# Moving the taps' subtraction of the maximum from VectorE to GpSimd

## The reference

```
w = exp(weight_gen - max over the 7 taps)          # [4, 4096, 8 heads, 7]
w = w / (sum over taps + 1e-9)
x1[s] = sum_k w[s, h, k] * x_pad[s + k]            # 192 channels, 24 a head; causal padding of 6
xn = x1 / sqrt(mean(x1^2) + 1e-6) * rms_g
out = (silu(xn @ w_gate) * (xn @ w_val)) @ w_out   # 192 -> 1536 -> 192, 16384 tokens
```

## Time and profile before

| | |
|---|---|
| median of 3 runs | 1322.19 us (1322.03 to 1322.69) |
| the profiled execution | 1322.03 us, span 1320.2 us |
| granted TensorE clock, mean | 0.992 of full speed |
| TensorE matmul busy | 1277.4 us (97%) |
| VectorE busy | 992.0 us (75%) |
| ScalarE busy | 662.8 us (50%) |
| GpSimd busy | 83.3 us (6%) |

### The profile page before, as it was taken

The page is one execution under the profiler, slowest core; times in us unless marked ns, Lnnn a source line. Parts: engine busy times, 40 slices in busy tenths (PEclk is TensorE's granted clock), DMA queues, the critical chain, the costliest instruction groups (busy, mean ns, idle before and its releaser), DMA issues.

```text
span 1320.2 us, 33644 instructions
## 1 busy us (share of the span) xinstructions
PE 1277.4 (97%) x13524; PEld 1260.1 (95%) x13524; DVE 992.0 (75%) x1441; ACT 662.8 (50%) x1427; POOL 83.3 (6%) x101
## 2 busy tenths in 40 slices
PE   3798999999999999999999999999999999999998
PEld 3687889999999999999999999999999999999998
DVE  6788877777777778777778777777777777777653
ACT  4364565445555445555444555444555444555543
POOL 7600000000000000000000000000000000000000
PEclk9799999999999999999999999999999999999999
DMA  9121211211221211221211221111121121121010
GB/s 307 38 67 27 65 58 52 67 56 37 67 67 43 67 55 37 67 67 43 67 55 41 63 67 48 62 55 56 47 67 60 50 67 55 37 67 37 14 37 13
DMA packets 20101, 77.69 MB, mean 59 GB/s; under 512 B 3215, under 2 KB 5007, under 8 KB 19854
## 3 DMA queue, kind: packets, MB, share of 16 engines
q1 hardware_dynamic: 19982, 75.83, 18.9%
HBM read 38.07 MB, written 12.58 MB: 38 GB/s over the span
## 4 chain that ended last, share of the span: by engine, by line
PE 89%; DVE 5%; issue 2%; ACT 2%; DMA 1%; POOL 0%; SPq 0%; POOLq 0%
PE up_ps L620 59%; PE out_ps L651 26%; PE out_ps L655 3%; DVE y L203 1%; DVE h L544 1%; DVE h_lo L562 1%; DMA xT<-xT 1%; DVE prod L201 1%; PE up_ps L588 1%; ACT taps L391 0%; ACT silu L410 0%; PE up_ps L592 0%; DMA taps<-in_weight_gen 0%; ACT h_hi L417 0%; DVE y L201 0%
## 5 line engine op out<-in xcount | busy, mean ns | idle before, releaser
L620 PE MATMUL up_ps<-xT,w_hi 64*128 64x512 f32 x4608 | 858.1, 396 | 14.9 <-DMA xT<-xT 6.5
L620 PEld LDWEIGHTS up_ps<-xT,w_hi 64*128 64x128 f32 x4608 | 627.3, 186 | 26.1 <-issue 8.1
L620 PE MATMUL up_ps<-xT,w_lo 64*128 64x512 f32 x2304 | 589.2, 395 | 0.0
L651 PE MATMUL out_ps<-wo,h_hi 64*128 64x384 f32 x3072 | 478.2, 354 | 3.1 <-issue 2.7
L655 PE MATMUL out_ps<-wo,h_lo 64*128 64x192 f32 x3072 | 453.3, 247 | 0.0
L544 DVE TENSOR_TENSOR h<-up_ps,silu 128x512 f32<-128x512 f32 x384 | 264.7, 689 | 234.1 <-ACT silu L410 233.8
L651 PEld LDWEIGHTS out_ps<-wo,h_hi 64*128 64x128 f32 x3072 | 425.8, 185 | 5.1 <-issue 3.9
L655 PEld LDWEIGHTS out_ps<-wo,h_lo 64*128 64x128 f32 x3072 | 421.2, 187 | 0.5
L417 ACT ACTIVATE h_hi<-h 128x512 fp32r<-128x512 f32 x384 | 242.7, 632 | 352.3 <-DVE h L544 292.0
L410 ACT ACTIVATE silu<-up_ps 128x512 f32<-128x512 f32 x384 | 228.7, 595 | 263.7 <-PE up_ps L620 259.5
L620 PEld LDWEIGHTS up_ps<-xT,w_lo 64*128 64x128 f32 x2304 | 349.5, 187 | 3.3
(11 more groups left out here) (43 smaller groups left out, 311.4 us busy)
## 6 DMA issues: line engine op xcount, KB each, us to landing
x_buf<-in_x SPq DMA_DIRECT2D x30, 960.0 KB, 4.5
xT<-xT SPq DMA_DIRECT2D x96, 256.0 KB, 3.8
result<-last SPq DMA_DIRECT2D x32, 384.0 KB, 2.3
taps<-in_weight_gen SPq DMA_DIRECT2D x1, 3248.0 KB, 19.5
raw<-in_moe_w_gate SPq DMA_DIRECT2D x3, 384.0 KB, 6.3
raw<-in_moe_w_val SPq DMA_DIRECT2D x3, 384.0 KB, 7.3
last<-in_moe_w_out SPq DMA_DIRECT2D x1, 1152.0 KB, 12.4
x_first<-in_x SPq DMA_DIRECT2D x2, 384.0 KB, 4.6
```

The source lines that it names most:

```text
L620: mm = nc.tensor.matmul(ps[:, banks, :], w[rows, s, cols], xT[rows, t, s, part, :], start=(s == 0 and n == 0), stop=ends)
L651: nc.tensor.matmul(out_ps[:, j, 0:2 * D], h_hi[rows, g % HB, cols], wo[rows, g, :, :].rearrange("p a d -> p (a d)"), start=(g == 0 and k < ...
```

## The change

The subtraction leaves VectorE and goes to GpSimd as `less_max`: piece 0 after GpSimd's convolution, piece 1 after `inverse_rms(2)`, piece 2 after `inverse_rms(3)`, each waiting for the maximum of its piece (`rest_max`). The maximum moves from behind h_lo of its block to directly behind h, before the block's mix steps. `steps_taps` is dropped, and tiles 1 and 2 use `steps_other`. `steps_first` has one step more in block 4 and one less in block 7. The exponential of tiles 1 and 2 goes from block 9 to block 8.

```diff
--- before.py
+++ after.py
@@ -317,8 +317,20 @@
                 pool.wait_ge(pool_mix, CONV + n)
                 conv_step(nc.gpsimd, n, x_first[:, J:PAD + 2 * J, :], tap_w1, y[:, 1, :, :], prod_pool).then_inc(pool_mix, 1)
 
-            for T in range(1, 5):
-                inverse_rms(T)
+            def less_max(n):
+                cols = pieces[n]
+                pool.wait_ge(rest_max, n + 1)
+                nc.gpsimd.tensor_tensor(taps[:, cols, :], taps[:, cols, :],
+                                        tap_max[:, cols].unsqueeze(2).to_broadcast([P, cols.stop - cols.start, K]),
+                                        ALU.subtract).then_inc(rest_less, 1)
+
+            less_max(0)
+            inverse_rms(1)
+            inverse_rms(2)
+            less_max(1)
+            inverse_rms(3)
+            less_max(2)
+            inverse_rms(4)
 
             def turn(i, last=False):
                 for t in range(2):
@@ -428,8 +440,8 @@
                             rest_exps(n)
 
             tile(0, 0, first=True, exps=((9, 0),))
-            tile(1, 1, exps=((9, 1),))
-            tile(2, 0, exps=((9, 2),))
+            tile(1, 1, exps=((8, 1),))
+            tile(2, 0, exps=((8, 2),))
             tile(3, 1)
             with act.Fori(2, TILES // 2 - 1) as i:
                 tile(2 * i, 0)
@@ -509,14 +521,6 @@
                     dve.wait_ge(taps_loaded, 16)
                 nc.vector.tensor_reduce(tap_max[:, pieces[n]], taps[:, pieces[n], :], AX_X, ALU.max).then_inc(rest_max, 1)
 
-            def rest_subtract(n):
-
-                dve.wait_ge(rest_max, n + 1)
-                cols = pieces[n]
-                nc.vector.tensor_tensor(taps[:, cols, :], taps[:, cols, :],
-                                        tap_max[:, cols].unsqueeze(2).to_broadcast([P, cols.stop - cols.start, K]),
-                                        ALU.subtract).then_inc(rest_less, 1)
-
             def out_add(T, t, stored):
                 dve.wait_ge(out_part_done, T + 1)
                 if stored is not None:
@@ -525,16 +529,13 @@
                 nc.vector.tensor_tensor(out_sb[:, t, :, :], out_ps[:, :, 0:D], out_part, ALU.add).then_inc(out_added, 1)
 
 
-            steps_first = [0, 0, 2, 2, 0, 2, 2, 2, 2, 2, 2, 1]
-            steps_taps = [2, 2, 2, 0, 2, 2, 2, 0, 2, 1, 1, 1]
+            steps_first = [0, 0, 2, 2, 1, 2, 2, 1, 2, 2, 2, 1]
             steps_other = [2, 1, 2, 2, 1, 1, 1, 1, 2, 1, 2, 1]
-            assert sum(steps_first) == sum(steps_taps) == sum(steps_other) == MIX
+            assert sum(steps_first) == sum(steps_other) == MIX
 
             def tile(T, t, i, first=False, mixes=True, last=False):
                 xf = turn_after(T)
-                tops = isinstance(T, int) and T < len(pieces)
-                steps = steps_first if first else steps_taps if tops else steps_other
-                max_at, subtract_at = (1, 4) if first else (3, 7)
+                steps = steps_first if first else steps_other
                 for f in range(FB):
                     b = pair(t, step_of(f, xf))
                     if f == 2 and not first:
@@ -544,6 +545,8 @@
                     nc.vector.tensor_tensor(h[:, f % 2, :], val_ps[:, b, :], silu[:, f % 2, :], ALU.mult).then_inc(h_done, 1)
                     if first and f == 0:
                         wo_low()
+                    if isinstance(T, int) and T < len(pieces) and f == (1 if first else 3):
+                        rest_maxima(T)
                     if mixes:
                         for n in range(sum(steps[:f]), sum(steps[:f + 1])):
                             if n == 0:
@@ -561,10 +564,6 @@
                     dve.wait_ge(h_hi_done, FB * T + f + 1)
                     nc.vector.tensor_tensor(h_lo[:, f % HB, :], h[:, f % 2, :], h_hi[:, f % HB, :].bitcast(F32),
                                             ALU.subtract).then_inc(h_lo_done, 1)
-                    if tops and f == max_at:
-                        rest_maxima(T)
-                    if tops and f == subtract_at:
-                        rest_subtract(T)
 
             tile(0, 0, 0, first=True)
             tile(1, 1, 0)
```

## The result

| | median | runs | ratio to before (95% interval) |
|---|---|---|---|
| before | 1322.15 us | 4 (1322.03 to 1322.69) | |
| changed | 1335.1 us | 4 (1332.93 to 1336.02); 15 in all, 1332.93 to 1337.96 | 1.0100 (1.0087 to 1.0113) |
| changed, on another chip (e8_after) | 1335.26 us | 4 | 1.0100 (1.0084 to 1.0117) |

The forecast was 1337.7 us. The profiled execution of the changed kernel took 1334.78 us, with a span of 1333.0. How much of the 13 us is the change's own is taken up behind the experiments: profiles that are alike in the opening differ by 10.6.

The account below looks back on a forecast made before the run. TensorE bounds the kernel. Tiles 1 and 2 each add 6.8 - 0.96 + 0.3 + 1.55 = 7.7 us, together 15.4, and tile 0 adds 0.3: 1322.0 + 15.7 = 1337.7 us, range 1329 to 1344.

Parts of the forecast that it names:

- TensorE sets the time and only tiles 0 to 2 count: From tile 3 on TensorE is busy throughout and unchanged; tiles 1 and 2 idle 3.63 and 3.59 us.
- GpSimd's subtraction stands in front of VectorE: Tiles 1 and 2: second mix step after the maximum blocked, about 6.7 us not 0.96; TensorE goes on 6.8 later.
- Its length: GpSimd's subtraction of 2688 elements in tiles 1 and 2: 5.9 us, with 4.9 and 6.4 kept as alternatives.
- fourth rival: Blocking as forecast, but clock stays up or GpSimd at 4.9: 1334.6, both 1332.6; counted within the forecast, chance 0.78.
- The waits behind it: Tile 1, TensorE's waits for h(5) and x_low, 0.17 + 0.79 = 0.96 us, go; tile 2 alike.
- The exponential: Moved to block 8: TensorE waits 2.2 us before the last block in place of 1.87, +0.3 a tile.
- The clock: Low level (1.2 GHz) after the long wait before block 5's projection, +1.55 us a tile in tiles 1 and 2.
- Tile 0: GpSimd's 1120 elements take 2.6 us and delay h_lo(3): +0.3 us, possibly up to 1.5 or nothing.
- work beside VectorE: Rival: GpSimd's subtraction runs beside VectorE in tiles 1 and 2, +0.4 us a tile, 1323; chance 0.10.
- the gain: Rival: no block, earlier h(8) shortens the exponential's wait and clock stays up at 128.09; about 1318, chance 0.05.
- dear rows of seven: Rival: rows of 7 cost GpSimd about twice as much, 5.9 us more each in tiles 1 and 2: 1349.5; chance 0.07.

Follow-up runs that it names:

- e8_after: Changed kernel, unedited, timed again on another chip beside the kernel before and the variants; 1335.26 us, ratio to before 1.0100.
- e2: Changed kernel with each of GpSimd's three subtractions cut to its first 224 elements a partition, order and waits unchanged; ratio to before 1.0004.
- e4: Kernel before with only the subtraction moved from VectorE to GpSimd; maximum, mix steps and exponential stay in place; ratio to before 1.0041.
- e5: Changed kernel with GpSimd's subtraction in 5, 12 and 12 instructions of 224 elements instead of three long ones; ratio to before 1.0007.
- e6: Changed kernel with a memset of the same taps, which only writes, in place of GpSimd's subtraction; 1323.24 us, one run.
- e7_same: Kernel before, unedited, run again for a second profile; 1324.16 us, one run.

## Why the prediction was right

- **TensorE sets the time and only tiles 0 to 2 count.** Right: from the addition at 194.45 to that at 234.01 tile 3 has no idle time.
- **GpSimd's subtraction stands in front of VectorE.** Right, to the instruction: second mix step after the maximum. e2, e4, e5 and e6 each take away one part of the mechanism (length, order, one long hold, reading) and the rows follow it.
- **Its length.** This was the mis-sized term. I took 5.9 us from the add; it held VectorE for 4.74, and 4.91 with its start (e4), which is the lower bound that I scaled from the product, 4.9. From h(3) to h(4) I had 108.42 - 96.75 = 11.67 us, measured 108.98 - 98.48 = 10.50; the difference of 1.17 is 5.9 - 4.74 within the rounding of the rows. (The fourth rival gives 1334.6 for a clock that stays up or for 4.9 us. It belongs to the clock; 4.9 alone makes it 1337.7 - 2.0 = 1335.7.)
- **The waits behind it.** 0.17 and 0.79 went, as forecast. The exponential: forecast 2.2, measured 2.07, +0.2 instead of +0.3. In sum 6.31 - 0.79 - 0.96 + 0.20 = 4.76 us a tile, which is the 4.75 of idle time in the windows.
- **The clock.** It fell after the long wait, in both tiles, as forecast. In busy time of TensorE tile 1 is 0.54 under before (41.28 against 41.82) and tile 2 1.43 over (42.03 against 40.60 from 137.99 to 182.18), where I had 1.55 over in each. Before paid for its own low clock in tile 1, which I had left in the sum, and the changed kernel had none behind its wait of 2.07 us (1.00 from 131.34 to 134.60). Tile 2 paid more than tile 1, since its low stretch reached about 5 us into the work instead of 3.24. Where such a stretch comes is not fixed: e2_short has 0.61 behind a wait of 2.00 us in tile 1 and 1.00 behind one of 1.97 in tile 2.
- **Tile 0.** Forecast +0.3. GpSimd's small subtraction took 2.16 us (forecast 2.6), and VectorE's L190 was held by it for 2.37 us instead of 0.39, but by e7_same tile 0 isn't longer (94.41 against 94.68).

Against e7_same, which has the same opening, the spans differ by 1333.0 - 1322.4 = 10.6 us: 4.2 in tile 1, 6.2 in tile 2, 0.3 in tile 3, -0.3 in tile 0. Twice 4.75 is idle time, the other 1 is busy time, most of it at the low clock. My sum had 15.7: 2.3 too much for the length, about 1.5 for the clock left in at the boundary of tile 1, 0.6 for tile 0, and 0.7 in small terms. So the working was 5 us too high, half as much again as the 10.6, while the median missed the forecast by only 2.6. That the number looks better than the working is luck: all four executions of before in the result lie near 1322 us, as the profiled one, which has no low clock in the opening, and the profiled one of the changed kernel has it. Over all 42 executions of before on record the median is 1324.0, over all 19 of the changed kernel 1335.2, 11.3 us apart (on several chips).

Of the rivals, work beside VectorE is out by the 5.53 us rows, the gain with it, and dear rows of seven by the 4.91. Not settled: whether the cheaper rate comes from the broadcast operand, which the product has too and the add has not, or from something else.

## What to carry to other kernels

Before moving work to GpSimd, look at what VectorE does meanwhile. In these runs an instruction with two inputs in SBUF waited until the end of a GpSimd instruction that reads, and the maximum over the taps (`TENSOR_REDUCE`) and an h with one input in PSUM kept their time. A single input is no safe sign, as the `TENSOR_SCALAR` below shows. Short instructions on GpSimd took most of the price away (e5_chunks). That a long one does no harm if the chain that TensorE waits for isn't queued behind it is my reading of these traces, and no run tests it: in e4_moved_only the wait went from h(4) to h(5) and stayed. Cutting and spreading VectorE's own work, without moving anything to another engine, won 0.61%, where the move with its instructions cut (e5_chunks) can't be told from before. Before crediting freed time on an engine, look at which wait ends last: the 7.2 us of waits in tiles 1 and 2, and the low clock behind them, were what there was to win there, and the freed 2.95 us stood in front of none of these waits.

## What the runs showed of the hardware

- A waiting engine got the memory at the end of the other's current instruction, ahead of the other's next one: in the changed kernel GpSimd got it at 102.90 us, between VectorE's two mix steps. In e5_chunks twelve GpSimd instructions took 10.62 us beside VectorE's, and the two mix steps and h_lo behind the maximum lasted 0.26 to 0.37 us longer each.
- One input in SBUF was not enough to be spared. Before, in the opening, a small VectorE instruction with one tensor input and a constant (`TENSOR_SCALAR`, 32 elements) took 1.21 us and ended 0.03 after GpSimd's add; the same one takes 0.18 us elsewhere. The maximum over the taps and an h from PSUM passed in their usual time (1.30 us for 1120 elements, 0.68 us).

```profile
54.50 1.21 DVE L187 TENSOR_SCALAR tap_sum<-tap_sum 128x32 f32<-128x32 f32 x1
```

```profile
53.83 1.85 POOL L203 TENSOR_TENSOR y<-y,prod_pool 128x768 f32<-128x768 f32 x1
```

- A memset of 2688 elements on GpSimd (2.35 us) and a two-input VectorE instruction ran side by side (0.96 us).
- GpSimd's subtraction with a broadcast operand took 4.91 us for 2688 elements, against 1.83 for an add of 768 with no broadcast.
- Before, the same wait of 1.87 us was followed by a granted clock of 0.51 at one tile boundary (from 128.09 us) and of 1.00 at the next (from 173.54).
